# Gated attention and two expert layers on one core: the tail of the first quarter reordered (flag, holes, gate piece, next alphas)

## The reference, cut to what matters

```python
def _attn_ref(q, k, v, alpha):            # 2 x 8 heads, 768 steps, 48 wide
    for t in range(S):
        state = alpha[:, :, t, :, None] * state + np.einsum('bhd,bhe->bhde', k[:, :, t], v[:, :, t])
        y[:, :, t] = np.einsum('bhd,bhde->bhe', q[:, :, t], state)
    return y

def _moe_ref(x, w_gate, w_val, w_out, rms_g):      # 1536 tokens, 384 -> 1536 -> 384
    rms = np.sqrt(np.mean(x * x, axis=-1, keepdims=True) + 1e-06)
    xn = x / rms * rms_g
    g = xn @ w_gate
    silu = g * (1.0 / (1.0 + np.exp(-g)))
    val = xn @ w_val
    return (silu * val @ w_out)

def _moe2_ref(x, domain_probs, w1, w2):            # 4 experts, 384 -> 1024 -> 384
    p = domain_probs / (domain_probs.sum(-1, keepdims=True) + 1e-09)
    for e in range(E):
        h = np.maximum(x @ w1[e], 0.0)
        out += p[:, e:e + 1] * (h @ w2[e])
```

## Time and profile before

| what | value |
|---|---|
| median of 3 runs | 702.3 us (702.28 to 702.66) |
| profiled execution, its own time | 702.73 us |
| span of its trace, first to last instruction | 700.7 us |
| TensorE busy | 686.8 us, 98% |
| VectorE / ScalarE / GpSimd busy | 462.5 / 259.2 / 320.4 us |
| chain that ended last, by engine | PE 91%, SPq 4%, DVE 3% |
| granted TensorE clock, mean over the span | 1.000 |

### The profile page before, as it was taken

One profiled execution on the slowest core, in us unless ns is written; L12 is line 12 of the kernel. 1 busy time (PEld: TensorE's weight loads), 2 busy tenths in 40 slices (PEclk: granted clock), 3 DMA queues, 4 the chain that ended last, 5 costly groups with the idle time before them and its releaser, 6 DMA issues.

```text
span 700.7 us, 10702 instructions
## 1 busy us (share of the span) xinstructions
PE 686.8 (98%) x4006; PEld 636.2 (91%) x4006; DVE 462.5 (66%) x809; ACT 259.2 (37%) x471; POOL 320.4 (46%) x401
## 2 busy tenths in 40 slices
PE   7799999999999999999999999999999999999998
PEld 6689999999999999998899999999999999999997
DVE  6976666655546543316858777877787779777876
ACT  3832324132522243227414344434343334433430
POOL 3378761121111114840294685558645765577200
PEclk9999999999999999999999999999999999999999
DMA  8894380005102000200001101110011101100003
GB/s 179 210 198 111 100 170 1 9 1 103 35 1 77 1 1 24 68 0 1 1 23 46 46 2 45 46 46 13 33 46 46 32 15 46 45 24 1 23 0 136
DMA packets 71748, 35.13 MB, mean 50 GB/s; under 512 B 53904, under 2 KB 70672, under 8 KB 71696
## 3 DMA queue, kind: packets, MB, share of 16 engines
q1 hardware_dynamic: 71696, 34.44, 19.4%
HBM read 31.48 MB, written 2.36 MB: 48 GB/s over the span
## 4 chain that ended last, share of the span: by engine, by line
PE 91%; SPq 4%; DVE 3%; issue 1%; ACT 0%; DMA 0%; ACTq 0%; DVEq 0%
PE out_ps L1335 13%; PE out_ps L1337 13%; PE out_ps L1336 13%; PE hid_ps L1328 7%; PE hid_ps L1330 7%; PE hid_ps L1329 7%; PE at_ps L1526 4%; PE at_ps L1525 4%; PE at_ps L1524 4%; PE hid_ps L1525 2%; PE hid_ps L1526 2%; PE hid_ps L1524 2%; PE at_ps L1378 2%; SPq L452 2%; PE at_ps L1392 1%; PE at_ps L1424 1%
## 5 line engine op out<-in xcount | busy, mean ns | idle before, releaser
L1210 DVE SCALAR_TENSOR_TENSOR x<-out_ps,prob,x 128x384 f32<-128x384 f32 x180 | 110.4, 614 | 58.7 <-PE out_ps L1337 58.7
L1335 PE MATMUL out_ps<-early_r,late_r 128*128 128x384 f32 x384 | 129.3, 337 | 0.3 <-DVE x L1210 0.3
L1336 PE MATMUL out_ps<-early_r,late_r 128*128 128x384 f32 x384 | 129.5, 337 | 0.0
L1337 PE MATMUL out_ps<-early_r,late_r 128*128 128x384 f32 x384 | 129.4, 337 | 0.0
L668 POOL TENSOR_TENSOR hid_lo<-act_sb,hid_hi 128x384 fp32r<-128x384 f32 x44 | 44.8, 1019 | 169.5 <-ACT hid_hi L853 169.4
L909 ACT COPY late<-at_ps 128x512 f32<-128x512 f32 x98 | 57.7, 588 | 108.0 <-PE at_ps L1526 105.2
L1175 DVE TENSOR_TENSOR act_sb<-hid_ps,act_sb 128x384 f32<-128x384 f32 x48 | 26.6, 555 | 81.1 <-PE hid_ps L1330 71.1
L1335 PEld LDWEIGHTS out_ps<-early_r,late_r 128*128 128x128 f32 x384 | 72.2, 188 | 6.6 <-DVE x L1210 0.9
L1336 PEld LDWEIGHTS out_ps<-early_r,late_r 128*128 128x128 f32 x384 | 72.1, 188 | 5.2
L1337 PEld LDWEIGHTS out_ps<-early_r,late_r 128*128 128x128 f32 x384 | 72.2, 188 | 0.0
L722 POOL TENSOR_TENSOR early<-stage 128x128 f32<-128x128 f32 x14 | 6.5, 462 | 129.8 <-PE at_ps L1526 102.8
(11 more groups left out here) (260 smaller groups left out, 1614.2 us busy)
## 6 DMA issues: line engine op xcount, KB each, us to landing
stage<-in_moe_w_dram SPq DMA_DIRECT2D x32, 384.0 KB, 3.3
alpha_all<-in_alpha_dram SPq DMA_DIRECT2D x8, 288.0 KB, 5.2
stage<-in_moe_w_out_dram SPq DMA_DIRECT2D x4, 576.0 KB, 3.9
out_dram<-x SPq DMA_DIRECT2D x12, 192.0 KB, 1.9
stage<-in_moe_w_gate_dram SPq DMA_DIRECT2D x8, 216.0 KB, 4.1
stage<-in_moe_w_val_dram SPq DMA_DIRECT2D x8, 216.0 KB, 4.0
a_tm<-in_alpha_dram SPq DMA_DIRECT2D x9, 192.0 KB, 3.8
k_tm<-in_k_dram SPq DMA_DIRECT2D x9, 192.0 KB, 3.7
```

The lines of the kernel that those rows point to most:

```text
L1210: dve.scalar_tensor_tensor(out=a, in0=part, scalar=p, in1=a, op0=ALU.mult, op1=ALU.add).then_inc(s_acc, 1)
L1335: pe.matmul(dst, ah, bh, start=first, stop=False)
L1336: pe.matmul(dst, ah, bl, start=False, stop=False)
L1337: return pe.matmul(dst, al, bh, start=False, stop=last)
```

## The change

- In `FIRST`, `S 3` and `KS 3` come ahead of `E 4`.
- `SQD 2` (a square on VectorE) becomes `SQ 2` (on ScalarE), which waits for VectorE's two copies of that pair instead of ScalarE's.
- `NEXT 0` (VectorE's clamp of the next alphas) comes ahead of `N` (flag load and branch) and `XS`.
- SyncE issues piece 0 between alpha parts 4 and 5, and `next_a(1)` ahead of `fill_holes(0)`.
- Behind the sum of squares of quarter 0, TensorE's warming products are 2 instead of 4.

```diff
-                                            "TQ 3", "E 3", "M 2", "M 3", "Y 1", "S 2", "KS 2", "E 4", "S 3", "KS 3",
+                                            "TQ 3", "E 3", "M 2", "M 3", "Y 1", "S 2", "KS 2", "S 3", "KS 3", "E 4",
                                             "E 5", "KV 2", "ST 2", "KV 3", "ST 3", "E 6", "YD 2", "E 7", "SQ 1",
-                                            "YD 3", "SQD 2", "W 0", "SQD 3", "N 0", "XS 0", "NEXT 0", "SS 0", "R 0"))]
+                                            "YD 3", "SQ 2", "W 0", "SQD 3", "NEXT 0", "N 0", "XS 0", "SS 0", "R 0"))]
...
             load_alphas(4)
+            load_piece(0)
             load_alphas(5)
             load_alphas(6)
             load_alphas(7)
-            load_piece(0)
             load_piece(1)
             rows_to_lanes(sp, gcol[:, :].rearrange("p (j n) -> p j n", n=1), rms_g.rearrange("(r n) -> r n", n=1),
                           s_small, True)
+            next_a(1)
             fill_holes(0)
-            next_a(1)
             load_piece(2)
...
                 elif name == "SQ":
-                    act.wait_ge(s_yc, 2 * f + 2)
+                    if f == 2:
+                        act.wait_ge(s_yd, 2)
+                    else:
+                        act.wait_ge(s_yc, 2 * f + 2)
                     act.wait_ge(s_hole, 96)
                     squares(PAIR_ORDER[f])
...
                     mm.then_inc(s_ss, 1)
                     if i == 0:
-                        keep_warm(4)
+                        keep_warm(2)
```

## The result

The changed kernel is slower. Its median is 706.04 us against 702.79 of the kernel before on the same chip (16 runs each); the ratio is 1.0044, with a 95% interval from 1.0034 to 1.0053. That is outside the range of the prediction and on the other side of no change: 3.3 us later instead of 1.1 earlier.

What follows compares the result with a forecast made beforehand. TensorE, busy 98% of the 700.7 us span, was taken as the bound, so only the first gate product's start could move: 38.72 to 37.6, 1.1 earlier, giving 701.2 us from a 702.3 median, range 700.2 to 702.9.

Steps and rivals of the forecast that it cites:

- part 2: Holes on SyncE: issued behind three alpha issues costing 2.00 and a 0.04 gap, the last lands at 33.68 instead of 31.64.
- Rival C: Holes queue behind the alphas: landing 36.9, first gate product 40.3, time 703.9, slower; chance 0.12.
- Part 1: Flag on VectorE: without the square ahead of it, done at about 32.6 instead of 33.76, 1.1 earlier.
- part 4: Early gate piece: GpSimd's val split ends by 34.4 to 35.5, before xn_lo; later alpha parts hidden by 1.7.
- Part 3: From holes to first gate product: three xn_lo take 1.7 if GpSimd is idle, 3.43 if not; start 37.6 or 39.3.
- Part 5: Behind the first gate product: 0.95 of VectorE is freed, but TensorE's stream has no gap, so nothing counted.
- the sum's last line: First gate product 1.1 earlier carries to the end: span 699.6, and the same 1.1 off the median gives 701.2.
- Rival D: Gain swallowed at the second val piece, split 1.37 before use: gain above 1.4 stops; another such wait 702.0 to 702.4; chance 0.08.

Runs made afterwards that it cites:

- experiment 1: Changed kernel with the six hole transfers issued ahead of the next alphas again; 702.34 us, ratio 0.9989 to the kernel before.
- 4: Changed kernel with SyncE waiting, ahead of the next alphas, until quarter 0's states are done; 706.56 us, ratio 1.0050 to the kernel before.
- experiment 2: Kernel before with one line moved: the next alphas issued ahead of the holes; 706.25 us, ratio 1.0040.
- experiment 3: Changed kernel with the four gcol transfers issued behind the holes instead of ahead of the next alphas; 706.88 us, ratio 1.0044 to the kernel before.
- 5: Changed kernel with only two of eight heads of the next alphas ahead of the holes, the rest behind; 702.94 us, ratio 1.0013 to the kernel before.
- Experiment 7: Changed kernel with 27 instead of 6 warming products ahead of the sum of squares; 704.64 us, ratio 1.0031 to the kernel before.
- experiment 6: Changed kernel with 19 instead of 6 warming products ahead of the sum of squares; 704.27 us, ratio 1.0014 to the kernel before.
- 10: experiment 1 with the prob transfer moved from ahead of piece 3 to behind the next quarter's v; 701.15 us, ratio 0.9977 to the kernel before.
- 11: experiment 1 with prob late, the clamp back behind XS, and hid_lo of f = 1 on VectorE; 700.58 us, ratio 0.9970 to the kernel before.
- experiment 9: Kernel before with only SQ 2 on ScalarE, its wait, and KS 3 ahead of E 4, no transfer moved; 702.51 us, ratio 1.0010.
- experiment 8: experiment 1 with the first gate piece back behind alpha part 7; 702.40 us, ratio 0.9992 to the kernel before.

## Why the prediction was wrong, point by point

**The step that failed is part 2, "2.00 and a gap of 0.04".** It took the issue time of the alphas from the place where it was measured, behind the holes, and carried it 4.3 us forward. There it was 6.69. The price of an issue is not a property of the transfer: 2.02 at the end of the val piece, whose last transfer was still to land (experiment 1), 1.82 with nothing on its way (4), 4.44, 6.69 and 7.63 with more of the pieces outstanding (2, the changed kernel, 3), and 1.46 at the same early hour for a quarter of the bytes (5). The kernel before had a row that warned of it. Behind the next alphas and a weight piece of 576 KB, three transfers of 192 KB each, of the same form as the alphas, took 3.70 to issue there, single ones up to 1.77:

```profile
33.41 3.70 SPq L452 DMA_DIRECT2D k_tm<-in_k_dram  x3
```

The holes, last issued at 35.48 instead of the forecast 31.13, then landed in 1.86, better than the 2.55 taken. Rival C had the right place and sign, but put its price into the landing (5.8) and not into the issue, and gave all of it 0.12. It set the landing at 36.9 and G0 3.4 behind it. The landing was 37.34, and G0 came 5.17 behind it, 1.77 more than the rival had. VectorE kept the rival's pace (`xn_lo` was ready 3.33 behind the landing); it is TensorE that was late, by the 1.70 of the slow SS.

**The clock was not in the sum.** Rival C had TensorE ready to go as soon as the landing came. TensorE had stood for 3.79 by then, and SS took 1.70 more. Experiment 7 shows the size in its rows; experiment 6 shows, in one execution, that warming products that end 2.0 too early can be wasted.

**Part 1, the flag, held.** In the changed kernel's trace it was done at 33.46, 0.3 ahead of the 33.76 of before and not 1.1. TensorE's excess sum waited for the last alpha check, which ended at 32.80 instead of 31.86, because ScalarE had waited 0.94 for an earlier alpha part at 22 us; part 4 had looked only at the last part's cover ("hidden by 1.7"). But no other trace has this wait, also where the order ahead of the flag is the same: in experiments 1, 4, 7, 10 and 11 the flag is done at 32.48 to 32.52 (forecast 32.6), and only in 5 and 6 late again, at 33.32 and 33.04, without that wait. So the lateness is a matter of the execution and not shown to be one of the order. In experiment 9, with the gate piece in its old place, the flag alone brought G0 1.44 earlier.

**Part 3 and part 4 held in the main.** The three `xn_lo` took 1.68 in the changed kernel (forecast 1.7), and 3.16 where the val split was still going (experiment 8; 3.43 in the earlier trace rows). The Trainium skill's "SBUF — State Buffer", section "Who interferes with whom", says that such VectorE and GpSimd instructions exclude each other for their whole length; the rows of `xn_lo` agree. The clamp, with one input, was slower beside a split too: 0.95 with GpSimd idle, 1.73 and 1.57 in experiments 1 and 8. The gate split started at 26.47. The val split ended at 35.95, later than the 34.4 to 35.5 of the forecast, since it could start only at 31.77 and not by 31.3; it was still over before `xn_lo`. With the holes first G0 was at 37.43, forecast 37.6, but this closeness is in part luck (experiment 1).

**Part 5, "I count nothing", and the sum's last line, were wrong in a way that the result hides.** "699.6, the same 1.1 earlier" assumed that TensorE's stream behind G0 has no wait because it shows none. A stream without a wait can still have a place without slack. O1 had one of 0.06 (52.56 to 52.62). With the stall removed G0 came when it was forecast, and the time still was 702.34 and not 701.2. Rival D named the mechanism, but took the first piece whose slack it had looked up (1.37, second val piece) and not the tighter one before it.

**What stays open.** Which of the queue's resources is full while SyncE blocks was not tried. The DMA engines are not idle in the stall: from 25 to 29 us their mean share is 1.08 to 1.29 in every microsecond, and only from 29 to 30 is it 0.20. So the work still ahead on them is a candidate. Busy engines alone don't make the stall, though: from 25 to 28 their share is 1.08 to 1.12 in experiment 1 too, where the small holes go out in 3.75. Experiments 3 to 5 show that the stall goes with the unfinished transfers ahead and with the amount of the new ones; they don't show whether one engine's part of the work, the bytes or a count of rows is what fills up.

The stall's length varies. The same list of SyncE gave 6.69, 7.14 and 5.80 in the traces of the changed kernel and of experiments 6 and 7. Its end goes with the landing of the val piece's last transfer in all five traces that have a stall: it ended at 31.47, 29.51, 29.55, 32.17 and 30.57 (changed kernel, experiments 2, 3, 6, 7), and the landings were at 31.7, 29.8, 29.8, 32.4 and 30.7. So most of the 2.25 between experiment 2 and the changed kernel goes with the earlier landing of that piece. Which of the two sets the other, and why it landed earlier, isn't shown. Stalls above 4.44 were only seen with the gate piece moved up.

## What to carry to other kernels

A large transfer of many short rows, issued while others are unfinished, can hold its whole issuing queue for microseconds, so small transfers that someone waits for go ahead of it; and an issue time read behind them is no price for the place ahead. Before a gain at one point is passed on to the end, look through the engines behind it for the next consumer with no slack (an operation that ends just when its reader starts), above all where its start hangs on a landing that the gain doesn't move. If a wait for TensorE becomes longer than it was, or moves to another place, look at the granted clock behind it. And before a wait seen in one execution is called a cost of the change, look for it in a second trace with the same order.

## What the hardware showed unexpectedly

- Three transfers of 192 KB each took 1.82 to 7.63 us to issue on SyncE, by what was outstanding, and one single issue up to 4.97 (experiment 3).
- A landing can be fast behind a slow issue: the last hole took 1.86 from issue to landing after a stall of 6.69, and 2.55 when it stood behind no stall. It isn't a rule: in experiment 2 it took 3.05 behind a stall of 4.44.
- After 3.79 us without a product TensorE ran SS at half its clock, although it had been at the full one before; after 2.00 us behind 38 warming records it did so too, in one execution (3.57 for SS), while a stretch of 1.12 busy us in three (experiment 3) was followed by three whole microseconds at 0.50. Shorter stands did it in single executions: 1.46 ahead of O1 (experiment 9) and 2.12 ahead of G0 (experiment 8). The 1.26 and 0.99 of experiment 1 did not.
